# Attention heads regrouped from pairs of 64 rows to threes of 40 rows in an mLSTM and expert kernel

## The reference, cut to what matters

```python
batch, n_heads, seq, head_dim = (2, 8, 768, 40)        # attention; C and n start at zero
for t in range(S):
    m_new = np.maximum(f_gate[:, :, t] + m, i_gate[:, :, t])
    f_stab = np.exp(f_gate[:, :, t] + m - m_new)
    i_stab = np.exp(i_gate[:, :, t] - m_new)
    C = f_stab[:, :, None, None] * C + i_stab[:, :, None, None] * np.einsum('bhd,bhe->bhde', vt, kt)
    n = f_stab[:, :, None] * n + i_stab[:, :, None] * kt
    h_tilde = np.einsum('bhde,bhe->bhd', C, qt)
    denom = np.maximum(np.abs(nq), 1.0)                 # nq = n . qt
    y[:, :, t] = sigmoid(o_gate[:, :, t]) * h_tilde / denom
x = y.transpose(0, 2, 1, 3).reshape(1536, 320)
x = leaky(x @ w_in) @ w_out                             # 320 -> 2048 -> 320
P = sinkhorn(exp(x @ w_gate))                           # 8 experts
out = sum over e of P[:, e:e + 1] * (relu(x @ w1[e]) @ w2[e])   # 320 -> 1024 -> 320
```

## Time and profile before

| what | value |
| --- | --- |
| time of 3 runs | median 1006.07 us, from 1004.85 to 1007.33 |
| the profiled execution | 1007.05 us, with a span of 1005.3 us from its first to its last instruction |
| PE busy | 978.7 us of the span |
| DVE, ACT, POOL busy | 411.3, 296.5 and 72.6 us |
| mean granted TensorE clock | 0.992 of full speed |
| exponents of unit 4 start on PE | at 52.19 us |
| the last score matmuls of unit 11 start | at 110.40 us |

### The profile page before, as it was taken

The page is one execution under the profiler, slowest core; times in us unless marked ns, Lnnn a source line. Parts: engine busy times, 40 slices in busy tenths (PEclk is TensorE's granted clock), DMA queues, the critical chain, the costliest instruction groups (busy, mean ns, idle before and its releaser), DMA issues.

```text
span 1005.3 us, 14926 instructions
## 1 busy us (share of the span) xinstructions
PE 978.7 (97%) x5397; PEld 864.4 (86%) x5408; DVE 411.3 (41%) x784; ACT 296.5 (29%) x553; POOL 72.6 (7%) x146
## 2 busy tenths in 40 slices
PE   7699999999999979999999999999999999999998
PEld 5689988888778869998899999989998999899887
DVE  4546755546543364234244233324423332442222
ACT  4456444434432321123122121212212121321111
POOL 4335200000000322000000000000000000000000
PEclk9989999999999999999999999999999999999999
DMA  9774300210030002003001200300210030000000
GB/s 115 164 107 61 115 1 1 67 48 1 1 115 1 1 23 94 1 0 115 1 0 32 83 1 0 115 0 0 64 51 0 0 115 0 0 0 0 26 26 26
DMA packets 68462, 39.47 MB, mean 39 GB/s; under 512 B 52496, under 2 KB 64560, under 8 KB 68432
## 3 DMA queue, kind: packets, MB, share of 16 engines
q1 hardware_dynamic: 68256, 38.98, 16.3%
q10 hardware_dynamic: 176, 0.10, 0.0%
HBM read 36.91 MB, written 1.97 MB: 39 GB/s over the span
## 4 chain that ended last, share of the span: by engine, by line
PE 93%; SPq 4%; DVE 1%; DMA 1%; issue 0%; ACT 0%; DVEq 0%
PE psA L1108 44%; PE psB L1146 11%; PE psB L1148 11%; PE psB L1147 11%; PE psB L1124 2%; PE psB L1126 2%; PE psB L1125 2%; PE psB L1026 2%; PE psA L1003 1%; PE psB L1131 1%; PE psB L1130 1%; PE psA L996 1%; PE psB L1013 1%; SPq L288 1%; PE psB L1038 1%; SPq L328 1%
## 5 line engine op out<-in xcount | busy, mean ns | idle before, releaser
L659 ACT ACTIVATE gh<-psA 128x512 fp32r<-128x512 f32 x192 | 114.9, 598 | 538.1 <-PE psA L1108 538.1
L885 DVE SCALAR_TENSOR_TENSOR gl<-psA,gh 128x512 fp32r<-128x512 f32 x192 | 132.9, 692 | 340.9 <-ACT gh L659 340.7
L1146 PE MATMUL psB<-w2s,gh 128*128 128x320 f32 x768 | 237.6, 309 | 0.0
L1147 PE MATMUL psB<-w2s,gh 128*128 128x320 f32 x768 | 237.3, 309 | 0.0
L1148 PE MATMUL psB<-w2s,gl 128*128 128x320 f32 x768 | 237.2, 309 | 0.0
L1108 PE MATMUL psA<-xh,w1h 128*128 (+1 forms) x480 | 190.5, 397 | 0.0
L1108 PE MATMUL psA<-xl,w1h 128*128 (+1 forms) x480 | 189.8, 395 | 0.0
L1108 PE MATMUL psA<-xh,w1l 128*128 (+1 forms) x480 | 189.1, 394 | 0.0
L1147 PEld LDWEIGHTS psB<-w2s,gh 128*128 128x128 f32 x768 | 144.3, 188 | 5.5
L1146 PEld LDWEIGHTS psB<-w2s,gh 128*128 128x128 f32 x768 | 144.2, 188 | 5.1
L1148 PEld LDWEIGHTS psB<-w2s,gl 128*128 128x128 f32 x768 | 144.4, 188 | 0.0
(11 more groups left out here) (150 smaller groups left out, 878.6 us busy)
## 6 DMA issues: line engine op xcount, KB each, us to landing
raw<-in_moe_w_dram SPq DMA_DIRECT2D x16, 640.0 KB, 8.3
raw<-in_moe_w_dram SPq DMA_DIRECT2D x8, 1024.0 KB, 5.3
raw<-in_moe_w_dram SPq DMA_DIRECT2D x16, 256.0 KB, 6.1
raw<-in_moe_w_out_dram SPq DMA_DIRECT2D x4, 640.0 KB, 9.3
raw<-in_moe_w_in_dram SPq DMA_DIRECT2D x2, 1024.0 KB, 6.0
qs<-in_q_dram SPq DMA_DIRECT2D x12, 160.0 KB, 3.3
ks<-in_k_dram SPq DMA_DIRECT2D x12, 160.0 KB, 4.0
vz<-in_v_dram SPq DMA_DIRECT2D x24, 80.0 KB, 3.8
```

The costliest lines, as they stand in the source:

```text
L659: act.activation(gh[:, f % RING, :], h_ps[:, f % HB, :], ACT.Relu).then_inc(ghi_ok, 1)
L885: dve.scalar_tensor_tensor(out=gl[:, f % RING, :], in0=h_ps[:, f % HB, :], scalar=0.0, in1=gh[:, f % RING, :].bitcast(F32), op0=ALU.max, o ...
L1146: pe.matmul(bank, gh[:, slot, cols], W2S[par][:, f, 0, :], start=first, stop=False)
L1147: pe.matmul(bank, gh[:, slot, cols], W2S[par][:, f, 1, :], start=False, stop=False)
```

## The change

Heads stand in groups of three (the last group has two), each head with 40 rows, so a group has 120 rows (GR) and there are 3 groups instead of 4 pairs. The tiles of values, weighted values and state are plain `[128, 8, 41]`, without blanks. The key of a single head is now made by a copy of the whole group's rows with a mask of ones and zeros as its scale (three masked copies on ACT), and the state's new part is added with the same mask (three `scalar_tensor_tensor` on DVE). `intra` runs with one head's 41 columns to a matmul pair in place of 96. `inter` and its sum are left out for chunk 0, whose state is zero, and the new state for the last chunk, which nobody reads. v is loaded by one transfer of all 8 heads. The loops over units on PE and DVE are written out.

```diff
-        qs = [asb(f"qs{j}", [P, H, DP], F32) for j in range(U_IT)]
+        qs = [asb(f"qs{j}", [P, NG * GH, D], F32) for j in range(U_IT)]
-        vz = [asb(f"vz{j}", [P, HP, 2, VP], F32) for j in range(U_IT)]
+        vz = [asb(f"vz{j}", [P, H, DV], F32) for j in range(U_IT)]
...
+        def group(x, g):
+            return x[:, g * GH:min((g + 1) * GH, x.shape[1]), :].rearrange("p h d -> p (h d)")
+        def group_cols(x, g):
+            return x[0:P, g * GH * DV:min((g + 1) * GH, H) * DV]
...
             def load_v(n):
-                sp.dma_start(vz[j][:, :, 0, 0:D], vv[:, :, 0, :]).then_inc(v_in[j], 16)
-                sp.dma_start(vz[j][:, :, 1, VS:VS + D], vv[:, :, 1, :]).then_inc(v_in[j], 16)
+                sp.dma_start(vz[j][:, :, 0:D], v[b, :, rows, :].rearrange("h s d -> s h d")).then_inc(v_in[j], 16)
...
+            pool.memset(head_mask[:], 1.0).then_inc(consts, 1)
+            where(head_mask, ALU.is_ge, 0.0, 0, -D)
+            where(head_mask, ALU.is_ge, 0.0, D - 1, D, -1)
...
             def pool_unit(n):
-                for e in range(2):
-                    last = pool.tensor_tensor(wv[b][:, :, e, 0:DV], ...)
+                pool.tensor_tensor(wv[b][:], vz[j][:], heads_of(rw_t[:, 1, :]), ALU.mult).then_inc(wv_done, 1)
...
             def qk_copies(i, j):
-                act.copy(qt[b][:], qt_ps)
+                act.copy(qt[b][0:GR], qt_ps[0:GR, 0:NG, :])
                 at_least(act, s_done, n)
-                act.copy(kt[0:DP, :, 0, :], kt_ps[0:DP])
-                act.copy(kt[DP:P, :, 1, :], kt_ps[DP:P]).then_inc(qk_done, 1)
+                for e in range(GH):
+                    ng = len(range(e, H, GH))
+                    last = act.activation(kt[0:GR, 0:ng, e, :], kt_ps[0:GR, 0:ng, :], ACT.Copy, scale=head_mask[0:GR, e:e + 1])
+                last.then_inc(qk_done, 1)
...
-            dve.memset(kt[:], 0.0).then_inc(kt_blank, 1)
...
             def sums(i, j):
+                if c == 0:
+                    dve.sem_inc(fin_step, 1)
+                    dve.tensor_copy(hh[:], heads(intra_ps)).then_inc(ysum_read, 1)
...
             def new_state(i, j):                        # DVE
+                if c == NC - 1:
+                    return
-                for e in range(2):
-                    last = dve.tensor_tensor(st[b][rows, :, e, 0:DV], sp_v[rows, :, e, 0:DV], sd[b][rows, :, e, 0:DV], ALU.add)
+                for e in range(GH):
+                    last = dve.scalar_tensor_tensor(out=st[b][0:GR, e:H:GH, :], in0=heads(state_ps)[0:GR, e:H:GH, :],
+                                                    scalar=head_mask[0:GR, e:e + 1], in1=sd[b][0:GR, e:H:GH, :],
+                                                    op0=ALU.mult, op1=ALU.add)
...
             def transposes(i, j):
-                    for g in range(HP):
-                        last = pe.transpose(dst[:, g, :], src[:, 2 * g:2 * g + 2, :].rearrange("p e d -> p (e d)"), ident[:])
+                    for g in range(NG):
+                        last = pe.transpose(dst[0:GR, g, :], group(src, g), ident[:])
...
             def inter(i, j):
+                if c == 0:
+                    return
-                for g in range(HP):
-                    pe.matmul(inter_ps[:, cols], qt[b][:, g, :], st[b][:, g, :, :].rearrange("p e v -> p (e v)"),
+                for g in range(NG):
+                    pe.matmul(group_cols(inter_ps, g), qt[b][0:GR, g, :], group(st[b], g)[0:GR], start=True, stop=True)
...
             def intra(i, j):
-                for g in range(HP):
-                    for e in range(2):
-                        last = pe.matmul(intra_ps[:, cols], ws[:, 2 * g + e, :], vz[jj][:, g, e, :],
-                                         start=e == 0, stop=e == 1)
+                for h in range(H):
+                    last = pe.matmul(intra_ps[:, h * DV:(h + 1) * DV], ws[:, h, :], vz[jj][:, h, :], start=True, stop=True)
...
             def new_state(i, j):                        # PE
+                if c == NC - 1:
+                    return
-                for g in range(HP):
+                for g in range(NG):
+                    last = pe.matmul(group_cols(state_ps, g)[0:GR], group(ks[jj], g), group(wv[b], g), start=True, stop=True)
...
-            with pe.Fori(1, NU // U_IT) as i:
-                for j in range(U_IT):
-                    pe_unit(i, j)
+            for n in range(U_IT, NU):
+                pe_unit(n // U_IT, n % U_IT)
```

More of the change, by code:

```diff
@@ L46, in build @@
     NU = NC * B
-    HP = H // 2
-    DP = 64
+    GH = 3
+    NG = (H + GH - 1) // GH
+    GR = GH * D
     DV = D + 1
-    VS = 48
-    VP = 2 * VS
     TB = 512
@@ L119, in asb @@
             return sb(name, shape, dt, attn)
-        qs = [asb(f"qs{j}", [P, H, DP], F32) for j in range(U_IT)]
-        ks = [asb(f"ks{j}", [P, H, DP], F32) for j in range(U_IT)]
-        vz = [asb(f"vz{j}", [P, HP, 2, VP], F32) for j in range(U_IT)]
+        qs = [asb(f"qs{j}", [P, NG * GH, D], F32) for j in range(U_IT)]
+        ks = [asb(f"ks{j}", [P, NG * GH, D], F32) for j in range(U_IT)]
+        vz = [asb(f"vz{j}", [P, H, DV], F32) for j in range(U_IT)]
         og = asb("og", [P, NU, DM], F32)
@@ L558, in _ @@
             for b in range(B):
-                for x in (wv, st):
-                    flat = x[b][:].rearrange("p g e v -> p (g e v)")
-                    last = act.copy(flat, zero1[:].to_broadcast(list(flat.shape)))
+                flat = st[b][:].rearrange("p h v -> p (h v)")
+                last = act.copy(flat, zero1[:].to_broadcast(list(flat.shape)))
             last.then_inc(blank, 1)
@@ L732, in _ @@
             dve.wait_ge(rw_tr, 1)
-            dve.tensor_copy(rw_t[:], rw_ps).then_inc(gates_ok, 1)
+            dve.tensor_copy(rw_t[:], rw_ps)
             dve.wait_ge(dec_tr, 1)
-            dec_all = dec_ps.rearrange("p (q e c) -> p q e c", e=2, c=NC)
-            for half in range(2):
-                rows = slice(half * DP, half * DP + DP)
-                last = dve.tensor_copy(decp[rows, :, :], dec_all[rows, :, half, :])
-            last.then_inc(gates_ok, 1)
-            heads = lambda x: x.rearrange("p (h v) -> p h v", v=VS)
+            dve.tensor_copy(decp[:], dec_ps).then_inc(gates_ok, 1)
+            heads = lambda x: x.rearrange("p (h v) -> p h v", v=DV)
             def weigh(i, j):
@@ L810, in _ @@
                 low_parts(0, j - 2)
-            with dve.Fori(1, NU // U_IT) as i:
-                for j in range(U_IT):
-                    dve_unit(i, j)
-                    low_parts(i, j - 2)
+            for n in range(U_IT, NU):
+                dve_unit(n // U_IT, n % U_IT)
+                low_parts(n // U_IT, n % U_IT - 2)
             sums(NU // U_IT, -1)
@@ L1002, in scores @@
                 for h in range(H):
-                    last = pe.matmul(s_ps[:, h, :], kt[:, h // 2, h % 2, :], qt[b][:, h // 2, :], start=True, stop=True)
+                    last = pe.matmul(s_ps[:, h, :], kt[0:GR, h // GH, h % GH, :], qt[b][0:GR, h // GH, :], start=True, stop=True)
                 last.then_inc(s_done, 1)
```

81 lines of the change are left out of this document (32 added, 49 removed).

## The result

The changed kernel took 997.21 us in the median of 4 runs (996.4 to 997.99), the kernel before 1006.24 us in 4 runs beside it: a ratio of 0.991 with a 95% interval of 0.9894 to 0.9926, so 9.0 us less. The forecast was 1001.5 us, with a range that ended at 997.8. The direction was right, the size about half of what was measured.

What follows compares the result with a forecast made beforehand. PE, busy in 97% of the span, was taken as the bound, waiting for DMA before 52 us. Units' 3.36 us plus the early 1.2 gave 4.6 less: 1001.5 us against the median of 1006.07, range 997.8 to 1004.6.

Steps and rivals of the forecast that it cites:

- in the shadow of `weigh`: PE's `inter` runs while DVE's `weigh` does, so from unit 5 on its saving of 0.22 us is lost.
- the rival of a cheap `intra`: Matmul spacing goes by moving columns, `intra` falls from 1.76 to 0.74 us; 3.6 us more gained, 998; chance 8%.
- the rival of instruction fetch: Four more written-out units on PE add fetches that share the DMA engines; a 9 us stall gives 1010.5; chance 5%.
- forecast 0.82 + 0.22: Unit 11: 0.82 us saved between transposes and scores, where ACT binds at 3.04, and 0.22 from `inter`.
- 0.10 more was forecast: Units 7 and 8: 0.22 us saved on PE less 0.32 for ACT's longer copies, together -0.10.
- From unit 5 on the forecast was 2.70: Units 5, 6, 9 and 10 save 1.76 us, units 7 and 8 -0.10, unit 11 0.82 and 0.22.
- the early part: SP's queue before unit 4's exponents: v's single transfer brings them forward by 1.2 us, from -1.5 to 2.6.
- the 0.5 for v's second transfer: Unit 4's second v transfer, right ahead of the exponent rows in SP's queue, goes: 0.5 us counted.
- unit 4 at full-clock price: Unit 4, after PE's wait, saves 0.66 us, counted at full clock though its matmuls run at a granted 0.66.
- The rival of the eaten gain: Full DMA, slower v rows or masked operations at high bounds leave 1.9 to 3 us, 1003.1 to 1004.2; chance 26%.

Runs made afterwards that it cites:

- a_filled: Changed kernel with 20 matmuls on constant data put ahead of unit 4's exponents, in PE's wait; median 996.16 us, ratio 0.9901.
- a_both_undone_filled: Changed kernel with q and k landing at a pitch of 64, v by two transfers, and 34 filling matmuls ahead of unit 4; 999.20 us, ratio 0.9932.
- b_written_out: Kernel before with only the loops over units 4 to 11 on PE and DVE written out; 1007.20 us, ratio 1.0005.
- b_filled: Kernel before with its loops written out and 36 filling matmuls ahead of unit 4's exponents; 1004.09 us, ratio 0.9979.
- a_v_48: Changed kernel with value rows at a pitch of 48 elements rather than 41; 999.46 us, ratio 0.9925.
- a_again: The changed kernel without an edit, run six more times; median 1000.27 us, ratio 0.9927.
- b_both: Kernel before with q and k landing packed and v in one transfer; 1003.12 us, ratio 0.9967.
- a_nothing_left_out: Changed kernel with `inter` and its sum for chunk 0 and the new state for the last chunk put back; 998.05 us, ratio 0.9924.

## Why the prediction was right or wrong

**What it had right.** `inter` lay in the shadow of `weigh` and its saving was lost. `intra` with 41 columns cost 1.71 us where it had cost 1.76, so the pace is that of the weight loads; the rival of a cheap `intra` is refuted. A unit in the middle is 6.75 long, forecast 6.80; the 0.05 is about the part left out of the sum, 120-column loads at 0.100 us a record rather than 0.108 (the new state took 0.60 for 6 records, not 0.65). That agrees with the Trainium skill (TensorE: Matmul & The Clock Gate, section LDWEIGHTS), by which the time of a load goes by its columns. DVE's adds took 0.81 (0.90 taken), ACT's masked copies 1.42 (1.60 taken), and neither held PE in the middle units; no table load came with them. The written-out loops are worth nothing, 1.0005 (0.9994 to 1.0015), so the rival of instruction fetch is not borne out. The section of the Trainium skill that the prediction cited against loops (Runtime: NRT & Kernel Launch, section Instruction fetch mechanics) has the stall only where the branch's target is not yet fetched, which the prediction left out; no run shows which was the case here. Unit 11 took 6.78 against 7.83 before, 1.05 less, with its `inter`; forecast 0.82 + 0.22. That agreement is luck: with before's missing matmul it is 1.26 less, since ACT, which was to hold the scores until 3.04 us after the transposes, let them start after 2.75 (98.71 to 101.46). Units 7 and 8 together took 14.37 against 14.54, 0.17 less where 0.10 more was forecast: ACT's q and k copies in unit 8 took 1.79 against 1.64 before, 0.15 more where 0.32 was taken; the other 0.1 of the difference is not explained. From unit 5 on the forecast was 2.70, the profile has 51.33 - 48.13 = 3.20, or 3.4 with the missing matmul.

**The step that failed: the early part, "the packets (160 bytes a head and row, as before) are as many, so the queue may only wait elsewhere".** It put the early part at 1.2, within -1.5 to 2.6. (The terms of the prediction, 0.5 and 0 less 1.6, give -1.1 for the low end; no row gives the other 0.4.) The profile has 4.7 at unit 4's start, 4.3 with the missing matmul, and the experiments give 3.1 to 3.3 (a_filled against a_both_undone_filled by ratio; exponent rows issued at 46.77 with both edits undone against 43.49). The profile's figure holds the scatter of the old kernel's own start too: with the same loads, the kernel before, b_written_out and b_filled issued these rows at 47.86, 46.27 and 47.71. Nearly as many packets of as many bytes took less time each, because q and k land next to each other in SBUF. I had looked at the landing pitch of v alone, for which a_v_48 shows no effect. The trace of before had rows that hint at the price. It has two kinds of transfer with the same 160-byte runs: q and k, which land at a pitch of 256 bytes, and the output gates, which land packed. Bytes moved, in 40 slices, of the kernel before, from 19 to 23 us (q, k, v) and from 30 to 33 us (output gates):

```profile
GB/s 237 222 192 211 227 224 218 219 168 157 143 138 149 127 139 142 131 157 154 146 144 136 159 144 134 144 293 131 134 123 131 125 112 126 130 139 146 136 144 138
...
GB/s 0 21 7 0 0 0 0 0 51 109 139 139 132 102 151 192 230 233 231 203 186 190 226 224 237 239 243 233 230 211 201 158 167 126 137 166 188 220 231 224
```

and of the changed kernel from 19 to 22 us, q and k now packed:

```profile
GB/s 237 235 215 205 213 175 147 117 130 98 111 181 224 215 211 211 181 173 186 201 216 209 226 226 224 224 211 203 199 203 184 201 196 198 192 205 203 188 194 175
```

Some 140 GB/s over most of the stretch in which q, k and v land at their pitches, 230 at best for the packed gates; and about 200 once q and k are packed. The contrast isn't clean: the first eight slices of the first row, before the rate falls, have 192 to 237. Two units' q and k stood ahead of the weights in a full queue, and unit 4's own behind them, 0.33 MB each: at 230 in place of 140 GB/s that is 3 x (2.3 - 1.4) = 2.7 us, by an estimate in hindsight, and 2.1 at the 200 that the changed kernel then showed. From rows of before, that sum would have put the early part near 3, with the 0.5 for v's second transfer.

**The second step: unit 4 at full-clock price.** The prediction counted 0.66 for unit 4, on the ground that a stretch of low clock ends at about the same time. It doesn't end at a set time: the same kernel had 8.28 and 11.89 us for this unit. In the first profile that gave 1.22 less than before, in the second 2.4 more, and the times follow: the first four runs of the changed kernel ended by 997.99, the six of a_again reached 1001.57; of all ten the median is 998.0. That is a spread of some 4 us in one kernel which no view of a single profile shows. The price itself was right: at a clock of 1.00 the unit took 6.9 us in b_filled and 6.2 in a_filled, 0.7 less. So chance has a part in how far off the forecast was. By the ratio of a_again, 0.9927, the changed kernel stands at 998.9 us beside a kernel before of 1006.24, inside the forecast's range of 997.8 to 1004.6; the first four runs, at granted clocks of 0.990 and 0.991, had a median just below it. The early part was too small by 2 us in either case.

**The rival of the eaten gain** is refuted: the DMA queue gained time, and v's narrower rows cost none.

**Left open.** The two transfers don't add up in the starts: each undone alone in the new kernel costs 0.7 and 1.2 us at the issue of unit 4's exponent rows, both undone 3.3. In the times of the old kernel they do: the ratios fell by 0.0010 and 0.0024 alone and by 0.0033 together. And why both together in the old kernel (b_both) still left the k transfer of unit 4 2.3 us later than in the changed kernel was not found.

## What to carry to other kernels

A transfer's price isn't its bytes and packets alone: look at how its runs land in SBUF, and price a changed layout by the GB/s of whichever transfer in the trace already lands that way. Where an engine comes out of a long wait for data, don't put the work behind it at full-clock price and don't trust one profile of it; fill the wait with idle matmuls that end just before the data arrives, or price both clocks. And check how many instructions each record stands for before you subtract two starts. And when a wait is moved forward, look up what stands one unit behind it before counting the gain: here the next exponent rows and ACT's table loads took back two thirds.

## What the runs showed of the hardware that was not expected

- 160-byte runs that land packed, 320 float32 elements to a partition, took 14.9 to 15.2% of 16 DMA engines over the span, those at a pitch of 256 bytes 16.1 to 16.6% (18 profiles): 12 us of all 16 engines for 12 units' q and k.
- After a wait of 4.92 us PE's granted clock was 0.50, 1.2 GHz of 2.4, and the low stretch ended within the unit (8.28 us at a mean of 0.74). In another execution of the same kernel, after a wait of 6.83 us, it lasted all of the unit's 11.89 us. a_nothing_left_out had the short stretch after 8.02 us of waiting. With 20 matmuls of 512 columns in the wait, 4.48 us of work, it was 1.00 from the start.
- Plain float32 matmuls with weights of 128 columns took 0.107 us a record with 41 moving columns, 0.108 to 0.110 with 96 and 0.113 to 0.115 with 128; with weights of 120 columns and 123 moving columns it was 0.100.
